# A fused attention, dense and expert kernel: new orders at its two seams, and GpSimd computing the low parts of the last block's x1

## The reference

```python
# 1. windowed attention, chunks of 32 queries, 8 memory keys + 16 left + 32 own + 8 right
scores = scale * q_c @ k_full.T;  a = exp(scores - max);  out = (a / (sum(a) + 1e-9)) @ v_full
# 2. dense layer, w_in 512x2048, w_out 2048x512
h = x @ w_in;  g = h * cos(h);  x1 = g @ w_out
# 3. experts, 8 of them, w1 512x1024, w2 1024x512
do_compute = x1 @ w_skip > 0;  e = argmax(x1 @ w_gate);  gate = softmax(x1 @ w_gate)[e]
out = x1 + (do_compute) * gate * (relu(x1 @ w1[e]) @ w2[e])
```

## Time and profile before

| | us |
|---|---|
| median of three runs | 860.64 |
| the three runs | 859.3 to 861.66 |
| the profiled execution | 860.12 |
| its span, first to last instruction | 858.5 |
| PE / DVE / ACT / POOL busy in it | 820.1 / 512.7 / 464.1 / 82.5 |

### The profile page before, as it was taken

How to read it: one execution, slowest core, us unless ns; L and a number is a source line. 1 busy time by engine, 2 the same in 40 slices (tenths; PEclk the granted TensorE clock), 3 DMA queues, 4 the chain that set the end, 5 groups by cost and what they waited for, 6 DMA issues and landing times. The chain is left out here.

```text
span 858.5 us, 19371 instructions
## 1 busy us (share of the span) xinstructions
PE 820.1 (96%) x8088; PEld 724.2 (84%) x8088; DVE 512.7 (60%) x1045; ACT 464.1 (54%) x819; POOL 82.5 (10%) x108
## 2 busy tenths in 40 slices
PE   5799999999999999999999999999998999999994
PEld 4688888888888888888888888888896889999993
DVE  4577655555565556455555555564546777865551
ACT  3577765565564556655555655574445555554430
POOL 2000000010001001000100010010211622111000
PEclk9899999999999999999999999999999999999998
DMA  7942031103220420321032204101008598555200
GB/s 258 340 135 78 25 112 63 63 25 115 76 69 11 153 75 26 112 63 63 26 111 71 64 17 149 49 2 74 2 12 289 198 382 305 207 191 211 110 14 27
DMA packets 40033, 93.87 MB, mean 109 GB/s; under 512 B 6559, under 2 KB 6559, under 8 KB 39936
## 3 DMA queue, kind: packets, MB, share of 16 engines
q1 hardware_dynamic: 35968, 86.01, 28.5%
q0 software_dynamic: 3968, 6.52, 2.4%
HBM read 78.16 MB, written 17.00 MB: 111 GB/s over the span
## 5 line engine op out<-in xcount | busy, mean ns | idle before, releaser
L856 PE MATMUL h_ps<-xT_hi,in_hi 128*128 128x384 f32 x512 | 181.2, 354 | 1.4 <-DVE xT_lo L1239 1.4
L856 PE MATMUL h_ps<-xT_hi,in_lo 128*128 128x384 f32 x512 | 173.0, 338 | 0.0
L856 PE MATMUL h_ps<-xT_lo,in_hi 128*128 128x384 f32 x512 | 172.5, 337 | 0.0
L870 PE MATMUL y_ps<-out_hi,g_hi 128*128 128x512 f32 x384 | 151.4, 394 | 7.4 <-DVE g_lo L1344 7.4
L870 PE MATMUL y_ps<-out_hi,g_lo 128*128 128x512 f32 x384 | 152.6, 397 | 0.0
L870 PE MATMUL y_ps<-out_lo,g_hi 128*128 128x512 f32 x384 | 152.0, 396 | 0.0
L1056 ACT ACTIVATE hs<-h_ps 128x384 f32<-128x384 f32 x128 | 62.3, 487 | 155.4 <-PE h_ps L856 155.4
L1338 DVE TENSOR_SCALAR whole<-us 128x384 f32<-128x384 f32 x128 | 45.8, 358 | 135.4 <-ACT us L1057 133.6
L1080 ACT ACTIVATE us<-us 128x384 f32<-128x384 f32 x128 | 67.2, 525 | 85.4 <-DVE us L1340 85.1
L856 PEld LDWEIGHTS h_ps<-xT_hi,in_hi 128*128 128x128 f32 x512 | 96.7, 189 | 4.5 <-DVE xT_lo L1239 1.6
L856 PEld LDWEIGHTS h_ps<-xT_lo,in_hi 128*128 128x128 f32 x512 | 97.0, 189 | 1.5
(11 more groups left out here) (184 smaller groups left out, 1277.8 us busy)
## 6 DMA issues: line engine op xcount, KB each, us to landing
raw_a<-w SPq DMA_DIRECT2D x32, 512.0 KB, 7.4
raw_b<-w SPq DMA_DIRECT2D x32, 512.0 KB, 7.0
k_sb<-qk SPq DMA_DIRECT2D x22, 512.0 KB, 4.6
v_sb<-v SPq DMA_DIRECT2D x22, 512.0 KB, 3.6
x_mid<-x SPq DMA_DIRECT2D x24, 256.0 KB, 4.6
out<-x SPq DMA_DIRECT2D x24, 256.0 KB, 4.9
q_sb<-qk SPq DMA_DIRECT2D x22, 256.0 KB, 3.2
in_raw<-w_in SPq DMA_DIRECT2D x4, 1024.0 KB, 6.1
```

The costliest lines, as they stand in the source:

```text
L856: last = pe.matmul(h_ps[:, f % 2, 0:BN], w[:, dc, f * P:(f + 1) * P], x[:, half, dc, :], start=(n == 0), stop=(n == 3 * DC - 1))
L870: last = pe.matmul(y_ps[:, j, :], g[:, f % RING, j * P:(j + 1) * P], w[:, f, :], start=(f == 0 and n == 0), stop=(f == FT - 1 and n == 2))
```

## The change

- `ATTENTION`: the step "sum" moves from site b + 3 (before `fraction`) to b + 4 (behind g_low).
- The prologue gets an order of its own for each engine, x alternates between two banks, and TensorE does 3 products of the identity with itself after values(2) and 6 after x(2) (`keep_running`).
- SP: v(2) before w_in(0), w_out(0) right behind it; w_in(1) waits for the third values. The six clearing DMAs and all loads of `lists` move from GpSimd to SP; so does the wait for the last scatters.
- GpSimd: the memsets of xg[1] and xg[2] wait for the last g_lo, and GpSimd computes x1_lo = x1 - x1_hi, three tiles, ahead of its last `sort`.
- Seam: turning slot 0's rows goes between down(14) and down(15); the three transposes run without logits between them; ScalarE takes the middle copy; the logits share one bank which VectorE reads in place; 4 filler products before and 4 after `ranks`; the one-hot rows are made of x1_hi and x1_lo in fp32r, high parts first.
- The first expert product of slot 0 (`first_up`) starts on the halves of the rows as they come. VectorE's and ScalarE's orders follow, and rows_high(1), rows_low(1) go ahead of the last two w1 splits.

```diff
@@ -39,7 +39,7 @@
...
 for _j, _b in enumerate((5, 13, 21)):
-    ATTENTION += [(_b, "scores", _j), (_b + 1, "exp", _j), (_b + 3, "sum", _j), (_b + 4, "probs", _j),
+    ATTENTION += [(_b, "scores", _j), (_b + 1, "exp", _j), (_b + 4, "probs", _j), (_b + 4, "sum", _j),
                   (_b + 6, "values", _j), (_b + 8, "x", _j)]
...
@@ -47,9 +47,12 @@
...
-PROLOGUE = [("scores", 0), ("scores", 1), ("exp", 0), ("exp", 1), ("probs", 0), ("sum", 0), ("scores", 2), ("exp", 2),
-            ("sum", 1), ("values", 0), ("probs", 1), ("sum", 2), ("x", 0), ("values", 1), ("w_in", 0), ("probs", 2),
-            ("x", 1), ("w_in", 1), ("values", 2), ("x", 2), ("w_in", 2)]
+PROLOGUE_PE = [("scores", 0), ("scores", 1), ("probs", 0), ("values", 0), ("scores", 2), ("x", 0), ("probs", 1),
+               ("values", 1), ("probs", 2), ("x", 1), ("values", 2), ("x", 2)]
+PROLOGUE_ACT = [("exp", 0), ("probs", 0), ("exp", 1), ("x", 0), ("probs", 1), ("exp", 2), ("probs", 2), ("x", 1),
+                ("w_in", 0), ("x", 2), ("w_in", 1), ("w_in", 2)]
+PROLOGUE_DVE = [("scores", 0), ("scores", 1), ("sum", 0), ("values", 0), ("scores", 2), ("x", 0), ("sum", 1),
+                ("values", 1), ("sum", 2), ("values", 2), ("x", 1), ("w_in", 0), ("x", 2), ("w_in", 1), ("w_in", 2)]
 AHEAD = 3
...
@@ -482,11 +489,11 @@
...
             load_v(1, flat(v_pre[:, 0]), pre_v_ld[0])
+            load_v(2, flat(v_pre[:, 1]), pre_v_ld[1])
             load_in(0)
-            load_v(2, flat(v_pre[:, 1]), pre_v_ld[1])
-            sp.wait_ge(v_full, 2)
+            load_out(0)
+            sp.wait_ge(v_full, 3)
             load_in(1)
-            load_out(0)
             load_qk(3, flat(q_sb), flat(k_sb), qk_ld)
...
@@ -501,6 +508,16 @@
...
+            sp.wait_ge(ready, 5)
+            for n in range(6):
+                sp.dma_start(lists.rearrange("(n p r) c -> n p (r c)", n=6, p=P)[n, :, :],
+                             empty[:, :].bitcast(F32)).then_inc(emptied, 16)
+            def load_list(s, landed):
+                sp.dma_start(listed[:, s, :, :], lists[s * N:s * N + SLOT, :].rearrange("(a p) c -> p a c", p=P)
+                             ).then_inc(landed, 16)
...
@@ -521,8 +538,25 @@
...
+                    sp.wait_ge(h_full, (BLOCKS - 1) * FT)
+                    for n in range(BT):
+                        sp.wait_ge(pairs_st[n], 16 * (BLOCKS - 1))
+                    carry(sp)
+                    load_list(0, list_ld[0])
...
+            def load_lists():
+                for n in range(BT):
+                    sp.wait_ge(pairs_st[n], 16 * BLOCKS)
+                sp.wait_ge(xg_ld[0], 32)
+                carry(sp)
+                for s in (1, 0, 2):
+                    load_list(s, list_ld[s])
+                for s in range(3, E):
+                    load_list(s, lists_ld)
...
@@ -531,6 +565,8 @@
...
+                    load_lists()
                     sp.wait_ge(xg_ld[1], rows_landed(1))
...
@@ -645,10 +675,6 @@
...
                       allow_small_or_imprecise_dtypes=True).then_inc(ready, 1)
-            for n in range(BT):
-                pool.wait_ge(pairs_st[n], 16 * (BLOCKS - 1))
-            carry(pool)
-            load_list(0, 0, list_ld[0])
             pool.wait_ge(ready, 7)
...
@@ -659,15 +685,14 @@
...
                       allow_small_or_imprecise_dtypes=True).then_inc(ready, 1)
+            pool.wait_ge(glo_done, BLOCKS * FT)
             pool.memset(xg[1][:, :, :].rearrange("p a d -> p (a d)"), 0.0).then_inc(ready, 1)
             pool.memset(xg[2][:, :, :].rearrange("p a d -> p (a d)"), 0.0).then_inc(ready, 1)
+            for j in range(BT):
+                pool.wait_ge(x1hi_done, j + 1)
+                pool.tensor_tensor(x1_lo[:, j, :], x1[:, j, :], x1_hi[:, j, :].bitcast(F32),
+                                   ALU.subtract).then_inc(x1lo_done, 1)
             sort(BLOCKS - 1)
-            for n in range(BT):
-                pool.wait_ge(pairs_st[n], 16 * BLOCKS)
-            pool.wait_ge(xg_ld[0], 32)
-            carry(pool)
-            for s in (1, 0, 2):
-                load_list(s, s * N, list_ld[s])
             for n in range(BT):
...
@@ -888,55 +908,75 @@
             pe.wait_ge(ready, 2)
-            for step, j in PROLOGUE:
-                if step != "w_in":
-                    attend(-1, 1, step, j)
+            def keep_running(to, n):
+                for _ in range(n):
+                    pe.matmul(to, ident[:, :], ident[:, :], start=True, stop=True)
+            for step, j in PROLOGUE_PE:
+                attend(-1, 1, step, j)
+                if (step, j) == ("values", BT - 1):
+                    keep_running(turn[:, 0, 0:P], 3)
+                elif (step, j) == ("x", BT - 1):
+                    keep_running(turn[:, 0, 0:P], 6)
             blocks(pe, run)
             down(BLOCKS - 1, FT - 2)
-            down(BLOCKS - 1, FT - 1)
-            def last_turned(j):
-                pe.wait_ge(y_free, BT * (BLOCKS - 1) + j + 1)
-                for dc in range(DC):
-                    last = pe.transpose(last_turn[j][:, dc * P:(dc + 1) * P], x1[:, j, dc * P:(dc + 1) * P], ident[:, :])
-                last.then_inc(last_x1_full, 1)
-            def last_logits(j):
-                pe.wait_ge(last_x1_done, j + 1)
-                for dc in range(DC):
-                    for c in range(4):
-                        r = slice(dc * P + c * 32, dc * P + (c + 1) * 32)
-                        last = pe.matmul(last_lg[j][c * 32:(c + 1) * 32, :], x1T_last[:, j, r], wr[:, dc, :],
-                                         start=(dc == 0), stop=(dc == DC - 1))
-                last.then_inc(last_lg_full, 1)
-            last_turned(0)
-            last_turned(1)
-            last_logits(0)
-            last_turned(2)
-            last_logits(1)
-            last_logits(2)
             pe.wait_ge(xg_ld[0], 32)
-            pe.wait_ge(last_lg_done, BT)
             for dc in range(DC):
...
                               start=(dc % 2 == 0 and a == 0), stop=False)
+            down(BLOCKS - 1, FT - 1)
+            for j in range(BT):
+                pe.wait_ge(y_free, BT * (BLOCKS - 1) + j + 1)
+                for dc in range(DC):
+                    last = pe.transpose(last_turn[j][:, dc * P:(dc + 1) * P], x1[:, j, dc * P:(dc + 1) * P], ident[:, :])
+                last.then_inc(last_x1_full, 1)
+            def last_logits(j):
+                for dc in range(DC):
+                    for c in range(4):
+                        r = slice(dc * P + c * 32, dc * P + (c + 1) * 32)
+                        last = pe.matmul(last_lg[c * 32:(c + 1) * 32, j, :], x1T_last[:, j, r], wr[:, dc, :],
+                                         start=(dc == 0), stop=(dc == DC - 1))
+                last.then_inc(last_lg_full, 1)
+            pe.wait_ge(last_x1_done, 1)
+            last_logits(0)
+            pe.wait_ge(last_x1_taken, 1)
+            last_logits(1)
+            pe.wait_ge(last_x1_done, 2)
+            last_logits(2)
+            keep_running(y_ps[:, 1, 0:P], 4)
...
             ranks().then_inc(last_ranks_full, 1)
+            keep_running(y_ps[:, 1, 0:P], 4)
+            def last_rows(part, i, j, ends):
+                for dc in (2 * i, 2 * i + 1):
+                    c = (dc % 2) * SLOT
+                    last = pe.matmul(s_ps[:, i, c:c + SLOT], part[:, j, dc * P:(dc + 1) * P], hot[:, j, :],
+                                     start=False, stop=(ends and dc % 2 == 1))
+                return last
+            for j in range(BT):
+                pe.wait_ge(x1hi_done, j + 1)
+                pe.wait_ge(hot_done, j + 2)
+                last_rows(x1_hi, 0, j, False)
+            for j in range(BT):
+                last_rows(x1_hi, 1, j, False)
             for i in range(2):
...
                     if i == 0:
-                        pe.wait_ge(hot_done, j + 2)
-                    for dc in (2 * i, 2 * i + 1):
-                        c = (dc % 2) * SLOT
-                        last = pe.matmul(s_ps[:, i, c:c + SLOT], x1[:, j, dc * P:(dc + 1) * P], hot[:, j, :],
-                                         start=False, stop=(j == BT - 1 and dc % 2 == 1))
+                        pe.wait_ge(x1lo_done, j + 1)
+                    last = last_rows(x1_lo, i, j, j == BT - 1)
                 last.then_inc(xg_full, 1)
@@ -949,9 +989,34 @@
...
+            def first_up():
+                def products(w, x, dcs, first, ends):
+                    for f in range(2):
+                        for dc in dcs:
+                            last = pe.matmul(h_ps[:, 0, f * SLOT:(f + 1) * SLOT], w[:, dc, f * P:(f + 1) * P], x[:, dc, :],
+                                             start=(first and f == 0 and dc == 0), stop=(ends and f == 1 and dc == dcs[-1]))
+                    return last
+                pe.wait_ge(w1hi_done, 1)
+                pe.wait_ge(xghi_done, 1)
+                products(w1_hi, xgT_hi, (0, 1), True, False)
+                pe.wait_ge(xghi_done, 2)
```

(57 more changed lines are left out.)

71 lines of the change are left out of this document (33 added, 38 removed).

## The result

The changed kernel takes 845.04 us in the median of four runs (844.25 to 846.27), the kernel before beside it 860.93 (859.3 to 861.66): a ratio of 0.9819, 95% interval 0.9801 to 0.9838. So it is 15.9 us faster, where 11.05 were forecast and a time of 849.6; 845.04 lies under the range of 846.8 to 854.0. The direction was right, the size was not.

A forecast was written before the change was run, and what follows sets the result against it. TensorE, busy 96% of the span, was taken as the bound, gaining only where idle, at half clock or doing avoidable work. Prologue 1.0, clock 1.75, sum 4.0, seam 4.2 and tail 0.1 gave 11.05: median 849.6 us, range 846.8 to 854.0.

The forecast's parts named there:

- the four kinds of place named: Where TensorE idles or runs at half clock: the prologue, the clock falls, waits for g_lo, the seam between dense stage and experts.
- the replay: Prologue: new order stepped through with the old rows' durations, x(2)'s low part at 23.8 for 25.2; 1.0 us earlier taken.
- The rival in which the first fall stays: First up product: the clock still falls to half there, 1.75 us less gain, 851.3 us; chance 0.16.
- eaten by out_low and in_low: Dense blocks: out_low and in_low behind the moved sum take 3 us of its gain back, 852.6 us; chance 0.06.
- (e): Seam: one-hot rows as 24 fp32r products of 256 columns take 2.9 us, for 5.45 as 12 fp32 products.
- (g): Seam: rows_high(1) and rows_low(1) ahead of the last two w1 copies remove the 1.14 us hole at 689.03.
- a second chain: Slot 1's scatter, lists and gather decide from about 2.4 us a GpSimd subtraction or with slow list loads; 852.8 us, chance 0.12.
- slower than before: Seam: GpSimd subtractions at 9.3 us each would make the kernel 2.6 us slower, 863.3 us; chance 0.02.
- the term for `hot`: Seam: hot may be held beside GpSimd's subtractions until 662.7 at most, 0.3 us off the gain.
- (a): Seam: with GpSimd's memsets waiting for the last g_low, whole is not slowed and down(14) starts at 649.95 for 650.90.
- The rival that a fall in the thinner seam would cost as much: Seam: a clock fall there would cost as much as one at the first up product, 1.75 us; no chance of its own.
- edit "loads": Changed load order, with the six clearing DMAs moved from GpSimd to SP: no gain or loss forecast.

## Why the forecast was too small

**What bounds it: right.** TensorE's work is the same within 2 us, and all the gain came out of the four kinds of place named, and the end.

**Prologue, forecast 1.0, got 0.** The step that failed is the replay. It took the stall as a cost of at most 1 us, if it belonged to the place in the instruction stream. It does: it fell into scores(2), as named there, and took 1.65. The run with more fillers shows why it could not be dodged: a kernel that reaches the place sooner only waits longer. The replay also let the clock rise where it rose before (18.9); it rose at 22.1, so the transposes of x(1) took 1.09 where 0.63 had been put in.

**Clock, forecast 1.75, got 1.38 and 1.51.** The mechanism was right, as the run without fillers shows. The first part is a bit smaller, since the first up product still takes 2.42 and not 2.05. The 1.51 in the next stretch is no part of the forecast's 1.75. The second fall, to which no gain was given because its hole stays (2.29 us), did not come in this execution. It did in the second one of the changed kernel (35.4 to 38.8 us; fourth h 13.21 us behind the first, for 11.86 and, before, 13.37). Of the eleven profiles with fillers, the fall is missing in the eight whose clock last rose at 22.1 us or later, and there in the three where it rose at 20.8 to 21.7. So 1.5 of the 15.9 is not to be had in every execution. The rival in which the first fall stays is out.

**Sum, forecast 4.0, got 5.5.** Block 0 is right: 3.0 forecast, 2.95 measured. The six later blocks were priced at the idle time of the row, 0.16, and gave 0.42 each (0.37 by the run with the step put back). The idle time is only a part. TensorE's timeline at one of them, of the kernel before and then of the changed one:

```profile
250.84 0.34 PE L856 MATMUL h_ps<-xT_hi,in_lo 128*128 128x384 f32 x1
251.34 0.50 PE L870 MATMUL y_ps<-out_hi,g_hi 128*128 128x512 f32 x1 [0.17 <-DVE g_lo L1344]
251.68 0.40 PE L870 MATMUL y_ps<-out_lo,g_hi 128*128 128x512 f32 x1
```

```profile
244.58 0.33 PE L876 MATMUL h_ps<-xT_hi,in_lo 128*128 128x384 f32 x1
244.75 0.39 PE L890 MATMUL y_ps<-out_hi,g_hi 128*128 128x512 f32 x1
244.98 0.40 PE L890 MATMUL y_ps<-out_lo,g_hi 128*128 128x512 f32 x1
```

The starts lie 0.50 and 0.34 apart with the wait, 0.17 and 0.23 without: 0.44 more, where the row says 0.17. The products overlap (each takes 0.33 to 0.40 and starts 0.17 to 0.23 behind the one before), and a wait costs that overlap too. The bound of 4.2 above was too tight for the same reason. Nothing was eaten by out_low and in_low; that rival is out.

**Seam, forecast 4.2, got 3.54.** Right are (e), 3.14 for 2.9 and 5.45 before, as long as the clock stays up (with a fall 4.5 to 5.5), (g), the hole at slot 1 (1.14 to 0.30), and the price of a subtraction, 1.25 for 1.2, so the two rivals that hung on it (a second chain, slower than before) are out. The scatter did come later than the forecast had it, 17.5 us behind the last h for 16.8 before and 16.0 by the prediction's 663.6, since its release waits for the held VectorE chain; but turning slot 1's rows waits for nothing. Mis-sized was the term for `hot` held beside the subtractions: at most 0.3 forecast, 1.2 measured against the run with the subtractions on VectorE. I had looked at the one op that would run into their end, not at the chain of fifteen small ops before it, two of which were held 0.6 each. And (a) is real but fragile: in the changed kernel whole takes 0.36 and down(14) is reached with 0.33 of waiting for 1.27, yet with the memsets back in the old place it was just as good. The rival that a fall in the thinner seam would cost as much was named in one sentence, without a chance of its own: such a fall came in nine of eleven profiles, and cost 1.3 to 2.3. That this profile has none is luck.

On the held `hot` the Trainium skill, "GPSIMD Engine Reference", Key points, says that GpSimd contends with VectorE instructions in a 2-port mode or with two SBUF inputs. The rows agree as far as they go: the op with two SBUF inputs, place_e, 0.78, was held, and so was the one-input op gate_sum, 0.73, of which no row says whether it ran in such a mode. The reduce ahead of them, the reciprocal between them and the place_e op that has one of its inputs in PSUM (653.23) took their usual 0.18. And its section Engine selection, which gives two-input elementwise work to VectorE as about twice as fast, agrees: 1.90 for three there, 3.77 here. The sum by that page was the same as mine; what was missed is that the contention is a price on the path.

**Tail, forecast 0.1, got 3.85: the largest miss.** The forecast for the move alone was right (0.2 on the kernel before). The step that failed is that the prediction took the 3 us between branch and DRAIN and the DRAIN of 6 us as fixed, and put the edit "loads" at nothing. Taking 15 transfers from GpSimd shortened its DRAIN by 1.2, and its code by the length at which the pause of 2.5 to 2.9 us ahead of the DRAIN goes (250 and 248 recorded instructions with it, 242 and fewer without). Only with the pause gone does moving the wait pay its 2.5. I had read the pause off as a fixed price of the end, since VectorE has one too; a pause with no wait behind it should have been an unknown with a bound from nothing to 3. With the tail bounded at 0.2, all bounds on the good side add up to 14.3 us (846.3, where the prediction says 846.4), so 845.04 was out of reach of its own best case.

The terms that failed: tail +3.75, sum +1.5, clock +1.1, prologue -1.0, seam -0.7, and 0.1 in the slots. Together +4.8, which is 15.87 - 11.05. This is the account of the two profiled executions, and the one of the changed kernel had its clock up in both doubtful places, worth 1.5 and at least 1.3 us; the second profile of the same kernel, with both falls, took 847.05.

What stays open: why the clock falls in one execution in the seam and not in the next with the same 2.26 us of idling before it; which of a memset and `whole` is held, and why; and, at the end, which boundary the code of GpSimd crosses; the runs show only between which lengths it lies (242 and 248).

## What to carry to other kernels

Price a wait that recurs by the start-to-start time of the instructions around it, not by the idle time in its row; and ask of every instruction on the path what another engine is doing beside it, above all of a chain of small ones. The end of the program is part of the sum: a pause without a wait, or a DRAIN, is not a constant, and an edit that takes instructions or transfers off an engine can move it, so list the engine's count of both before and after.
